# The first run of experts chosen from 18 of 24 token groups, and the list of runs made behind the order of tokens

## The reference

```
def _moe2_ref(x, modality_id, w_gate, modality_bias, w1, w2):
    logits = x @ w_gate + modality_bias[modality_id]      # x [3072, 384], 8 experts
    e_idx = np.argmax(logits, axis=1)
    probs = softmax of logits                             # gate_w: the chosen expert's
    for e in range(E):
        mask = e_idx == e
        if not mask.any():
            continue
        h = np.maximum(x[mask] @ w1[e], 0.0)              # w1 [8, 384, 1024]
        out[mask] = gate_w[mask, None] * (h @ w2[e])      # w2 [8, 1024, 384]
```

## Time and profile before

| | |
|---|---|
| three runs | 1026.02, 1028.05, 1028.32 us; median 1028.05 |
| the profiled execution | 1025.24 us, its span 1023.5 |
| TensorE busy | 976.9 us, 95% of the span |
| chain that ended last | PE 87%, DVE 4%, ACT 3%, issue 2%, DMA 2% |
| VectorE, ScalarE, GpSimd busy | 70%, 56%, 9% |
| mean granted TensorE clock | 0.986 |

### The profile page before, as it was taken

The page is one execution under the profiler, slowest core; times in us unless marked ns, Lnnn a source line. Parts: engine busy times, 40 slices in busy tenths (PEclk is TensorE's granted clock), DMA queues, the critical chain, the costliest instruction groups (busy, mean ns, idle before and its releaser), DMA issues.

```text
span 1023.5 us, 19055 instructions
## 1 busy us (share of the span) xinstructions
PE 976.9 (95%) x6668; PEld 945.2 (92%) x6669; DVE 712.0 (70%) x1300; ACT 574.1 (56%) x1069; POOL 90.5 (9%) x149
## 2 busy tenths in 40 slices
PE   5899899999999999999999999999799999999996
PEld 3778798999999999999999999999799999999996
DVE  4666998988888988888988877877543333663332
ACT  6557886876777876777778765554022223222221
POOL 2000000000000000000000000000022222442221
PEclk9899999999999999999999999999989999999998
DMA  9702221222221221221131110000341111441110
GB/s 210 217 7 33 40 40 24 40 63 40 40 62 40 40 63 40 40 63 34 31 72 23 24 36 20 1 24 26 113 174 38 46 38 38 158 149 38 38 46 24
DMA packets 146228, 58.66 MB, mean 57 GB/s; under 512 B 131321, under 2 KB 140551, under 8 KB 146160
## 3 DMA queue, kind: packets, MB, share of 16 engines
q1 hardware_dynamic: 139056, 42.61, 17.3%
q0 software_dynamic: 3904, 10.44, 3.2%
q10 hardware_dynamic: 3200, 4.72, 1.2%
HBM read 48.21 MB, written 10.03 MB: 57 GB/s over the span
## 4 chain that ended last, share of the span: by engine, by line
PE 87%; DVE 4%; ACT 3%; issue 2%; DMA 2%; SPq 0%; POOL 0%; POOLq 0%; DVEq 0%; ACTq 0%
PE bank L1646 20%; PE bank L1627 19%; PE bank L1862 13%; PE bank L1873 11%; PE bank L1551 4%; PE bank L1590 4%; PE bank L1538 4%; PE bank L1592 3%; PE bank L1573 3%; PE bank L1492 1%; PE bank L1485 1%; DMA w_sb<-in_moe_w_dram 1%; PE bank L1844 1%; DMA xg<-x_rows,idx_in 1%; PE bank L1616 1%
## 5 line engine op out<-in xcount | busy, mean ns | idle before, releaser
L1862 PE MATMUL bank<-xg_t,w_sb 128*128 128x128 f32 x1296 | 151.6, 278 | 1.7 <-issue 1.7
L1862 PEld LDWEIGHTS bank<-xg_t,w_sb 128*128 128x128 f32 x1296 | 150.9, 194 | 2.0 <-issue 2.0
L1627 PE MATMUL bank<-x_hi,w_in_hi 128*128 128x384 f32 x384 | 140.8, 367 | 1.9 <-DVE x_lo L1086 1.9
L1646 PE MATMUL bank<-w_out_hi,g_hi 128*128 128x392 f32 x384 | 141.7, 369 | 0.0
L1646 PE MATMUL bank<-w_out_lo,g_hi 128*128 128x392 f32 x384 | 131.1, 341 | 0.0
L1646 PE MATMUL bank<-w_out_hi,g_lo 128*128 128x392 f32 x384 | 131.0, 341 | 0.0
L1627 PE MATMUL bank<-x_hi,w_in_lo 128*128 128x384 f32 x384 | 130.7, 340 | 0.0
L1627 PE MATMUL bank<-x_lo,w_in_hi 128*128 128x384 f32 x384 | 130.4, 339 | 0.0
L945 ACT ACTIVATE he<-bank 128x128 f32<-128x128 f32 x216 | 59.9, 277 | 107.2 <-PE bank L1862 103.8
L762 ACT ACTIVATE hid<-bank 128x384 f32<-128x384 f32 x128 | 62.2, 486 | 83.3 <-PE bank L1627 82.6
L949 ACT ACTIVATE o_sb<-bank,gate_now 128x384 f32<-128x384 f32 x27 | 15.7, 582 | 115.9 <-PE bank L1873 115.9
(11 more groups left out here) (288 smaller groups left out, 2115.7 us busy)
## 6 DMA issues: line engine op xcount, KB each, us to landing
w_sb<-in_moe_w_dram SPq DMA_DIRECT2D x8, 1536.0 KB, 7.2
ab<-in_a_re_dram SPq DMA_DIRECT2D x24, 192.0 KB, 2.9
ab<-in_a_im_dram SPq DMA_DIRECT2D x24, 192.0 KB, 3.2
x_rows<-x_sb ACTq DMA_DIRECT2D x8, 576.0 KB, 3.1
qk_raw<-in_q_dram SPq DMA_DIRECT2D x22, 192.0 KB, 3.3
qk_raw<-in_k_dram SPq DMA_DIRECT2D x22, 192.0 KB, 3.4
v_in<-in_v_dram SPq DMA_DIRECT2D x22, 192.0 KB, 2.8
w_out_sb<-in_moe_w_out_dram SPq DMA_DIRECT2D x4, 768.0 KB, 6.0
```

Source lines behind the costliest of these rows:

```text
L1627: last = mm(bank_h[f % 2][:, 0:TT], w[:, kk, f * P:(f + 1) * P], x[:, m % 2, kk], start=(kk == 0 and i == 0), stop=(kk == KD - 1 and i == 2))
L1646: last = mm(bank_x2[t][:, 0:DE], g[:, u % RING, f % QF, t * P:(t + 1) * P], w[:, f], start=(f == 0 and i == 0), stop=(f == FT - 1 and i == 2))
L1862: last = mm(bank_h[f % 2][:, 0:P], w1_sb[par][:, kk, f * P:(f + 1) * P], xg_t[:, kk], start=(kk == 0), stop=(kk == KD - 1))
```

## The change

1. VectorE finds in the last slot, at gap 24, the first expert with a token in the first 18 groups (`lead_expert`, eight instructions). TensorE adds one product of eight columns to `early_ranks` for it. The order of experts now starts at the leader and goes round (`turn_e`, `up_to_e`), so it is sure to be run 0.
2. SyncE loads the leader's weights once the last `hidden` is done, ahead of the waits for the list and the MLP's end.
3. VectorE takes the order of tokens over first and makes the list of runs behind it, with five more instructions. GpSimd gathers tile 0 before it waits for the list; ScalarE and TensorE wait for the list (`runs_ready`) instead of `order_done`. TensorE's wait still stands between its 7 and 22 idle products, now with two loads behind it.
4. Run 0 is taken out of the loops over pairs on TensorE and VectorE. The loops go over runs 1 and 2, 3 and 4, and so on; the number of pairs is half the number of runs, rounded down, at least one.

```
--- before
+++ after
+            def weights_in(par, e):
+                sp.dma_start(w1_sb[par][:], w1[e].rearrange("(k p) f -> p k f", p=P)).then_inc(w1_in[par], 16)
+                sp.dma_start(w2_sb[par][:], w2[e].rearrange("(k p) f -> p k f", p=P)).then_inc(w2_in[par], 16)
+            sp.wait_ge(h_ready, NT * FT)
+            sp.wait_ge(lead_ready, 1)
+            leader = sp.value_load(lead_i[0:1, 0:1], min_val=0, max_val=E - 1)
+            weights_in(0, leader)
             sp.wait_ge(runs_ready, 1)
             sp.wait_ge(second_done, NQ * NT)
             with sp.Fori(0, run_pairs) as i:
-                for par in range(2):
-                    run = bass.ds(2 * i + par, 1)
+                for par in (1, 0):
+                    run = bass.ds(2 * i + 2 - par, 1)
...
-            act.wait_ge(order_done, 1)
+            act.wait_ge(runs_ready, 1)
...
+                    if m == NT - 1 and g == LEAD_AT:
+                        lead_expert(straight, lead_ready)
...
             gather(0)
+            pool.wait_ge(runs_ready, 1)
+            tiles = pool.value_load(runs_i[0:1, TOTALS, 0:1], min_val=1, max_val=MAXT)
             pool.wait_ge(xg_turned, 1)
             gather(1)
...
+            straight(dve.tensor_copy(gate_slot[:], bank_y[:, GC:2 * GC]))
+            straight(dve.tensor_scalar(order_f[:], bank_y[:, 0:GC], float(N), None, ALU.add))
+            dve.tensor_copy(order[:], order_f[:]).then_inc(order_done, 1)
...
-            straight(dve.tensor_scalar(runs_f[:, TOTALS, 1:2], runs_f[:, TOTALS, 1:2], 2.0, None, ALU.add))
+            straight(dve.tensor_scalar(runs_f[:, TOTALS, 1:2], runs_f[:, TOTALS, 1:2], 1.0, 2.0, ALU.add, ALU.max))
...
             take_tokens(0)
+            run_tiles = dve.value_load(runs_i[0:1, RUN_TILES, 0:1], min_val=1, max_val=MAXT)
+            split_w2(0, 16, 1)
+            with dve.Fori(0, run_tiles) as j:
+                expert_tile(j)
...
             stay_awake(7)
-            pe.wait_ge(order_done, 1)
-            run_pairs = pe.value_load(runs_i[0:1, TOTALS, 1:2], min_val=1, max_val=(E + 1) // 2)
+            pe.wait_ge(runs_ready, 1)
+            run_pairs = pe.value_load(runs_i[0:1, TOTALS, 1:2], min_val=1, max_val=E // 2)
+            run_tiles = pe.value_load(runs_i[0:1, RUN_TILES, 0:1], min_val=1, max_val=MAXT)
```

More of the change, by code:

```diff
@@ L1212, in place_ranks, with lead_expert @@
                 then(dve.tensor_copy(slot_hi[:, a:b], part_i[:, a:b]))
+            def lead_expert(then, ready):
+                then(dve.tensor_scalar(turn_e[:], bank_a[:, GE * E:(GE + 1) * E], 1.0, None, ALU.min))
+                then(dve.tensor_tensor(turn_e[:], turn_e[:], iota_e[:], ALU.mult))
+                then(dve.tensor_reduce(lead[:], turn_e[:], AX_X, ALU.max))
+                dve.tensor_scalar(lead_i[:], lead[:], -1.0, float(E), ALU.mult, ALU.add).then_inc(ready, 1)
+                then(dve.tensor_tensor(turn_e[:], iota_e[:], lead[:].to_broadcast([P, E]), ALU.is_gt))
+                then(dve.tensor_scalar(turn_e[:], turn_e[:], -float(E), None, ALU.mult))
+                then(dve.tensor_tensor(turn_e[:], turn_e[:], iota_e[:], ALU.add))
+                then(dve.tensor_tensor(up_to_e[:], turn_e[:].rearrange("p (a e) -> p a e", a=1).to_broadcast([P, E, E]),
+                                       turn_e[:].rearrange("p (e a) -> p e a", a=1).to_broadcast([P, E, E]), ALU.is_ge))
             def gates(then, a, b):
@@ L1235, in slow_route @@
                 place_ranks(then, bank_a, 0, GE)
+                lead_expert(then, s_led)
                 dve.wait_ge(s_exped_all, 1)
@@ L1434, in _ @@
                               ).then_inc(runs_ready, 1)
[L1435 to L1440, removed]
-            run_pairs = dve.value_load(runs_i[0:1, TOTALS, 1:2], min_val=1, max_val=(E + 1) // 2)
+            dve.wait_ge(runs_ready, 1)
+            run_pairs = dve.value_load(runs_i[0:1, TOTALS, 1:2], min_val=1, max_val=E // 2)
             def take_tokens(t):
@@ L1700, in early_ranks @@
                 mm(bank_a[:, 0:GE * E], earlier[:], chosen[:, 0:GE].rearrange("p g e -> p (g e)"), start=True, stop=False)
-                mm(bank_a[:, 0:GE * E], ones[:], running[EARLY_AT][:, 0:GE].rearrange("p g e -> p (g e)"), start=False, stop=True
-                   ).then_inc(ready, 1)
+                mm(bank_a[:, 0:GE * E], ones[:], running[EARLY_AT][:, 0:GE].rearrange("p g e -> p (g e)"), start=False, stop=True)
+                mm(bank_a[:, GE * E:(GE + 1) * E], ones[:], running[EARLY_AT][:, GE], start=True, stop=True).then_inc(ready, 1)
             def slot(m):
@@ L1845, in turn_tokens, with expert_tile @@
                 last.then_inc(xg_turned, 1)
+            def expert_tile(par, loaded, nth, t):
+                pe.wait_ge(w1_in[par], loaded)
+                pe.wait_ge(xg_copied, at(t + 1))
+                for f in range(FET):
+                    pe.wait_ge(he_copied[f % 2], at(FET // 2 * t + f // 2))
+                    for kk in range(KD):
+                        last = mm(bank_h[f % 2][:, 0:P], w1_sb[par][:, kk, f * P:(f + 1) * P], xg_t[:, kk],
+                                  start=(kk == 0), stop=(kk == KD - 1))
+                    last.then_inc(he_ready, 1)
+                turn_tokens(t + 1)
+                pe.wait_ge(o_copied, at(t))
+                pe.wait_ge(w2_hi_ready, nth)
+                pe.wait_ge(w2_lo_ready, nth)
+                for f in range(FET):
+                    pe.wait_ge(he_hi_ready, FC * t + f // 2 + 1)
+                    pe.wait_ge(he_lo_ready, FC * t + f // 2 + 1)
+                    for n, (h, w) in enumerate(((he_hi, w2_hi), (he_hi, w2_lo), (he_lo, w2_hi))):
+                        last = mm(bank_x2[0][:, 0:DM], h[:, f], w[par][:, f], start=(f == 0 and n == 0),
+                                  stop=(f == FET - 1 and n == 2))
+                last.then_inc(o_ready, 1)
             stay_awake(22)
             turn_tokens(0)
+            with pe.Fori(0, run_tiles) as j:
+                expert_tile(0, 16, 1, j)
             with pe.Fori(0, run_pairs) as i:
-                for par in range(2):
-                    run = bass.ds(2 * i + par, 1)
+                for par in (1, 0):
+                    run = bass.ds(2 * i + 2 - par, 1)
                     run_tiles = pe.value_load(runs_i[0:1, RUN_TILES, run], min_val=0, max_val=MAXT)
```

76 lines of the change are left out of this document (33 added, 43 removed).

## The result

The changed kernel takes 1030.43 us (median of 10 runs, 1028.69 to 1032.87), the kernel before, run beside it, 1027.22 (10 runs, 1025.73 to 1028.73). The ratio is 1.0033 [1.0021, 1.0044], which is 3.4 us slower. A second comparison on another chip gave 1.0026 [1.001, 1.0042], 2.7 us. The forecast was 1031.3, slower by 3.3. Five executions in all, four of the kernel before and one of experiment 4, took 1105 us or more; they stand in no ratio.

A forecast was written before the change was run, and what follows sets the result against it. The prediction took TensorE to bound the kernel nearly throughout. It summed 1.3 (start of tile 0), 1.8 (fifth weight pair) and 0.2 (extra product) to 3.3 us, on the median 1028.05 giving 1031.3; range 1026.5 to 1034.0.

The forecast's parts named there:

- List ready, loads, start of the 22: Ahead of tile 0: VectorE's list ready at 736.1 us, two loads on TensorE 1.2, its 22 idle products start at 737.3.
- The clock falls in the idle stretch, and the idle products pay: TensorE before tile 0: 5.7 us without work drops the clock; the 2.7 us warming price moves to the 22 idle products.
- Turn to output products: Tile 0: output products start 6.9 us behind the end of TensorE's turn, with VectorE's split slightly the later of two.
- No stall from the second gather: GpSimd's gather for tile 1 meets VectorE's cast, yet its rows arrive when tile 1's turn wants them: cost 0.
- Term 1: Start of tile 0: its output products begin at 752.6 instead of 751.34 us, 1.3 later.
- Leader's instructions: VectorE's eight instructions in the last slot, 1.7 us in all, fit within 2.2 us of slack: cost 0, at most 0.5.
- the extra product: TensorE's added product of eight columns for the leader: 0.2 us, bounded by 0 and 0.28.
- Term 2: Last run: a fifth pair of weight loads, for a run that doesn't exist, delays gather 17 and its output products: 1.8 us.
- this rival: Extra pair hides: gather 17 shares DMA engines fairly, lands in time, and 1.8 us goes: +1.5, 1029.6 us; chance 0.20.
- The other side of the forecast: TensorE's clock holds through the idle stretch before tile 0: -1.2 us without the last-run stall (chance 0.15), +0.6 with (0.10).
- The locked GpSimd: Tile 0: the second gather is locked out through both halves of VectorE's split: 2.2 more, +5.5, 1033.5 us; chance 0.17.

The follow-up runs named there:

- run 0: No follow-up run: the kernel's first run of tiles, which uses the weights w1 and w2 of the leader, the expert put first; no time of its own.
- experiment 4: Changed kernel with the list of runs ahead of the order of tokens on VectorE again, beside TensorE's order products: 1022.27 us, ratio 0.9961 to the kernel before.
- experiment 3: Changed kernel with 31 idle products instead of 7 ahead of TensorE's wait for the list: 1027.41 us, ratio 1.0008 to the kernel before.
- the second trace: Changed kernel profiled again without edit, on another chip: 1030.15 us, ratio 1.0026 to the kernel before.
- experiment 6: Changed kernel with VectorE's split of the first run's w2 ahead of its copy of tile 0: 1029.21 us, ratio 1.0021 to the kernel before.
- experiments 2 to 4: Second: changed kernel with TensorE's 22 idle products ahead of its wait for the list, 1023.10 us, ratio 0.9965 to before; third and fourth have their own lines.
- experiment 9: Kernel before with a fifth pair of weight loads added, nothing else: 1028.44 us, ratio 1.0027 to the kernel before.
- experiment 1: Changed kernel without the fifth pair of weight loads, so four pairs: 1028.59 us, ratio 1.0020 to the kernel before.
- experiments 10 and 11: Changed kernel with list beside order products and four weight pairs: 1021.46 us, ratio 0.9941; the same with first w2 split before tile 0's copy: 1020.00, 0.9961.

## Why the prediction was right

The time was right within 1 us, and the sign. By its steps:

- **List ready, loads, start of the 22** (736.1, then 737.3). Measured 737.08 and 738.42, with the order's end 0.9 later than before: the list 6.1 us behind it, forecast 6.0, then 1.34 to the 22, forecast 1.2. Right.
- **The clock falls in the idle stretch, and the idle products pay** (5.7 us of nothing, 8.0 for the 22). Measured 5.89 and 7.52 (6.87 in the second trace). Right, a little too dear; experiment 3 gave 2.3 us for the clock where I had 2.7.
- **Turn to output products** (6.9, the split as bound). Measured 6.7 from the turn's end at 746.28 to 752.98. Right in size, wrong in the bound: the products ended at 752.63, the split at 752.1, and experiment 6 shows that the split cost nothing.
- **No stall from the second gather.** Right. Descriptors out at 749.63, forecast at the latest 3.6 us behind the turn's end, measured 3.35. The Trainium skill's rule (SBUF — State Buffer, "Who interferes with whom") agrees in this trace: 2.24 us beside the cast and into the difference, 1.05 without them.
- **Term 1**, the start of tile 0: +1.3 forecast, +0.7 and +0.1 in the two traces, so too dear. Mechanism shown by experiments 2 to 4: against the first trace moved idle products gain 5.6, warmth 2.3, the list beside 7.1 (5.0, 1.7 and 6.5 against the second).
- **Leader's instructions.** Cost 0, right: VectorE's last split ends at 707.5 and TensorE wants it at about 709.2. The 0.2 for the extra product no run parts from the rest.
- **Term 2**, the fifth pair: +1.8 forecast, at the gather of the last run. The mechanism is shown by experiment 9, and the size was too small: 2.8 us by the times, 3.1 by the span. The arrival, 1.9 us late there, was within my 1.5 to 2.6. I had left out that a wait of about 3 us there costs the clock as well, another 1.2. The traces of before had that lesson in them, and I used it for tile 0 only. By the rule in the Trainium skill (DMA: Bandwidth & Descriptors, "Queues, rings and completion order") that an engine goes round between its queues packet by packet, my estimate was that the gather would land in about 1 us. The traces have 6.3 to 8.0 from issue to landing behind the fifth pair, and in the changed kernel's none of its packets moved for the first 3.8 us, so this rival fell.
- **Not in the forecast.** The tiles go at 9.875 us for 9.855, all of it in the output products (4.19 for 4.17), in every kernel with the change and in none without: 0.5 us over 26 tiles. Why wasn't tried. And w2 of the last run lands 1.2 us later in some executions, which hides part of the fifth pair's cost: beside it the pair is worth 0.6 to 1.3 us (experiment 1) where alone it is worth 2.8. Nor did I forecast GpSimd's delay one run earlier, in the first trace.

So the match has luck in it. Terms of 0.1 to 0.7, 3.2 to 4.2 and 0.5 for the pace stand in the two traces for 1.3, 1.8 and 0.2, 4.4 and 4.8 us in all, 1.1 and 1.5 more than forecast. The medians differ by less, 2.7 to 3.4, because the three traces of the kernel before are all of its quicker executions (1025.2 to 1025.3, with medians of 1026.0 to 1027.2 and timed runs from 1023.3 to 1032.9); what its slower ones wait for, no trace here shows.

The other side of the forecast, that the clock holds, fell with the windows. The locked GpSimd fell at tile 0 with the gather's 2.24 us; in the first trace GpSimd was held up beside both halves of a split at another place, ahead of the last run, at a cost that I had not priced there.

## What to carry to other kernels

When a chain of small instructions is moved off a shared stretch, price what is queued behind its wait, the idle products too: here a list that had been hidden came to cost 7 us, more than the 6 that the early weights and run 0's own loop gave. With the list left in its place the change is 4 us faster than the kernel before (experiment 4), and 4 to 6 with four pairs of loads as well (experiments 10 and 11). Look at loops whose count was rounded up for weights that nobody reads; 3 MB beside a small gather cost 2.8 us. And where a new wait of TensorE is priced, add the clock: behind single waits of 1.8 to 3.4 us the 24 products were 0.9 to 1.6 us dearer.

## What the runs showed of the hardware

- A gather of 192 KB issued at the last run behind 3 MB of weights landed 6.3 to 8.0 us after its issue (6.0 behind 1.5 MB). Beside run 1's weights the third gather took 4.2 (kernel before, second trace) to 6.2 us (experiment 1). In a quiet stretch it was 3.1 us (experiment 1's first gather).
- Waits of 1.4 to 1.5 us at the last run left the 24 output products at 4.36 to 4.42 us. Single waits of 1.83 (experiment 6) to 3.4 us made them 5.3 to 6.0. Two waits behind each other made them 5.97 (1.83 and 0.67 us, experiment 4) and 7.16 (1.89 and 0.88).
- The same 1.5 MB weight load was taken up 10.3 to 10.6 us after its issue in nine traces, 11.6 to 12.2 in five, and nothing between; the five have a 16 KB fetch of instructions near its end.
- The same indirect DMA took 1.05 us on GpSimd without, 2.24 within, VectorE's cast and difference. A copy of 128 indices there took 0.21 us alone and 3.31 beside the difference.
